# Query tiles from the last to the first in a fused attention, mixture and gating kernel

## The chip, the cores and the metric

The kernel runs on one core of a Trainium2 chip. The metric is the device time of one execution in microseconds (us). PE is TensorE, DVE is VectorE, ACT is ScalarE, POOL is GpSimd, SP issues the DMAs.

## The reference

Eight batches of 576 rows. A linear attention with a normalisation gives x (576 x 512); then four experts of causal attention (head size 64), each weighted by a top-2 gate; then a gated MLP that mixes along the sequence.

```python
kv = einsum('bhsd,bhse->bhde', k, v)              # "kv"
out = einsum('bhsd,bhde->bhse', q, kv)            # "o", then / rms * g_norm -> x
q, k, v = x @ wq[e], x @ wk[e], x @ wv[e]         # "qk", "v"
a = softmax(causal(scale * q @ k.T))              # "s", "exp", "scale"
x2 = sum over the chosen e of w_e * (a @ v @ wo[e])   # "t", "pv"
h = gelu(x2 @ w_in);  u, v = halves of h          # "u", "h"
v_s = w_sg @ layernorm(v) * g_ln + b_sg           # "vs"
y = x2 + (u * v_s) @ w_out                        # "out"
```

## The kernel before

Every engine walks one list, PLAN[part], and does its share of each unit (kind, j) in that order. There is no scheduler: the order of the lists is the order on each engine. Part -1 prepares weights and x of batch 0; parts 0 to 7 each do a batch, with the first product (kv, qT, o, x) of the next batch inside. Part 0 also splits the weights into a high and a low half (kinds split, w2e, wsgT, wsgR, wout).

The 640 rows (576 and 64 of padding) are five tiles of 128. An attention step n is one query tile and one pair of experts: tile n // 2, pair n % 2, ten steps. A step is

- s: PE scores (scores, L905 on), to a wide PSUM slot (w0, w1), 64 to 576 keys; step tiles of 576 keys take both slots. Two maxima by DVE (maximum, L695) follow.
- exp: two exponentials by ACT (L581), one for each expert of the pair.
- scale: DVE (scale_probs, L701) takes row_eps, row_inv and multiplies probs, and takes the maxima of the next step in between.
- t, t2: PE transposes probs to the narrow slots t0, t1 (L941), ACT copies them to work (L596); of a tile of five key blocks the last two (t2) are copied by DVE (L837).
- pv: PE multiplies with vals (L957) to a slot of t2, t3; when the second pair is in, ACT copies the tile's result to yT (L600) and DVE makes its low half (L829).

A unit waits on PE until the slot's last user is drained (dst). qk and v units are 12 matmuls of a projection (split_product, L887): the copy of a qk unit goes through ACT (L565) and then DVE (L815), and only then is the slot drained. scores asks for the drained qk units of its queries and keys. v units are copied by ACT (L561). h is 6 matmuls; gelu on ACT (L608), the statistics (L732), normalise (L742) and vhat_low (L727) on DVE, ln_inv on POOL and vhat_high (L524) on ACT make the layer norm, five tiles in turn. u units (L887, copied by a gelu, L610) go to w0, w1, w0, w1 and ask for all of yT; vs needs all five vhat tiles.

Of the kernel before, what the change touches and what calls it, by code (L numbers as in the profile page):

```python
# [55 lines left out]
def moe_chain(nc, q, k, v, g_norm, w_gate, wq, wk, wv, wo, w_in, g_ln, w_sg, b_sg, w_out, out):  # L56
# [18 lines left out]
    QK_ORDER = (0, EP, 1, EP + 1)  # L75
# [5 lines left out]
              ("split", "wqk0"), ("o", 3), ("x", 1), ("split", "wqk2"), ("w2", 3), ("o", 4), ("x", 2), ("x", 3), ("x", 4)]  # L81
# [13 lines left out]
    def attention(late_qk, late):  # L95

        plan = []
        for m in QK_ORDER:
            plan += [("qk", (m, 0))] + late_qk.get(m, [])
        for n in range(N - 2):  # L100
            plan += [("s", n)] + [("scale", n - 1)] * (n >= 1) + [("t", n - 2)] * (n >= 2) + [("exp", n)]
            plan += (late.get(n, []) if n == 0 else []) + BETWEEN.get(n, []) + (late.get(n, []) if n > 0 else [])
            plan += [("pv", n - 3)] * (n >= 3)
        return plan + [("t", N - 4), ("scale", N - 3), ("s", N - 2), ("exp", N - 2), ("pv", N - 5), ("t", N - 3),
                       ("pv", N - 4), ("scale", N - 2), ("s", N - 1), ("exp", N - 1)]

    ATTENTION = attention({}, {})
# [5 lines left out]
    MLP += [("u", m) for m in range(FC)] + [("vs", m) for m in range(FC)]  # L113

# [3 lines left out]
    GATE_STEP = [1, 8]  # L118
# [18 lines left out]
    def score_slots(n):  # L137

        return [(("s", n), WIDE[n % 2])] if P * (n // 2 + 1) - PAD <= 512 else [(("s", n, a), WIDE[a]) for a in range(2)]

    def scores_at(n, a):

        K = P * (n // 2 + 1) - PAD
        units_ = score_slots(n)
        unit, slot = units_[a % len(units_)]
        return unit, slot, 512 * a if len(units_) == 1 else W_LO, K

    def units(part):

        turn, got = [ring_start(part)], []  # L150

        def ring(unit, among):
            if part < 0:
                got.append((unit, FIRST_SLOT[unit]))
                return
            got.append((unit, among[turn[0] % len(among)]))
            turn[0] += 1

        for kind, j in PLAN[part]:
            if kind == "s":  # L160
                got += score_slots(j)
            elif kind == "t":
                got += [(("t", j, a, 0), NARROW[a]) for a in range(2)]
            elif kind == "t2":
                got += [(("t", j, a, 1), NARROW[a]) for a in range(2)]
            elif kind == "pv":
                if j % 2 == 0:
                    ring(("y", j // 2), NARROW[2:])
            elif kind in ("split", "double", "exp", "scale", "gelu", "wout", "w2e"):
                pass  # L170
            elif kind == "w2":
                if j == 0:
                    got += [((kind, c), WIDE[c]) for c in range(EP)]
            elif kind == "kv":
                if j == 0:
                    ring(("kv", 0), NARROW[2:])
            elif kind in ("u", "vs", "woT"):
                got.append(((kind, j), WIDE[j % 2]))
            elif kind == "out_y":
                got.append((("out", j), WIDE[j % 2]))  # L180
            elif kind == "out_g":
                pass
            elif kind == "h" and j in H_SLOT:
                got.append(((kind, j), H_SLOT[j]))
            elif kind in ("v", "h", "wsgT", "wsgR") or (kind == "qk" and j[1] == 1):
                ring((kind, j), NARROW[2:])
            else:
                ring((kind, j), NARROW)
        return got

    with ExitStack() as ctx:
# [319 lines left out]
        def _(act):  # L511
            def body(part):
# [8 lines left out]
                def vhat_high(s):  # L521
                    act.wait_ge(ln_ready, count(part, NT, s + 1))
                    rows = slice(PAD if s == 0 else 0, P)
                    nc.scalar.activation(vhat[rows, HI, s, :], ln_tile[s % 2][rows, :], ACT.Copy).then_inc(vhat_hi, 1)  # L524

                for kind, j in PLAN[part]:
# [40 lines left out]
                    elif kind == "s":  # L567
                        for g, (lo, hi) in enumerate(GATES):
                            if j == GATE_STEP[g]:
                                act.wait_ge(gate_dif, count(part, 2, g + 1))  # L570
                                nc.scalar.activation(g_exp[:, lo:hi, :], g_dif[:, lo:hi, :], ACT.Exp).then_inc(gate_exp, 1)
                    elif kind == "exp":
                        if j >= 2:

                            for a in range(2):
                                u.wait_full(act, part, ("t", j - 2, a, 0))
# [8 lines left out]
                    elif kind == "t":  # L585
                        lo, hi = T_GROUPS[j // 2][0]
# [11 lines left out]
                    elif kind == "pv" and j % 2 == 1:  # L598
                        t = j // 2
# [28 lines left out]
        def _(dve):  # L628
# [4 lines left out]
            def body(part):  # L633
# [18 lines left out]
                def gate_ranks(lo, hi):  # L652
# [3 lines left out]
                    u.wait_drained(dve, part, ("v", hi - 1))  # L656
# [44 lines left out]
                def scale_probs(n, maxima_of=None):  # L701

                    t, e = n // 2, n % 2
                    for g, (lo, hi) in enumerate(GATES):
                        if t == lo and e == 0:
                            gate_weights(g, lo, hi)
# [16 lines left out]
                def vhat_low(s):  # L723
                    dve.wait_ge(vhat_hi, count(part, NT, s + 1))

                    rows, dst = (slice(PAD, P), vhat[0:PAD, HI, 0, :]) if s == 0 else (slice(0, P), vhat[:, LO, s, :])
                    nc.vector.tensor_tensor(dst, ln_tile[s % 2][rows, :], as_f32(vhat[rows, HI, s, :]),  # L727
# [23 lines left out]
                for kind, j in PLAN[part]:  # L751
# [55 lines left out]
                    elif kind == "v":  # L807
                        for lo, hi in GATES:
                            if j == hi - 1:
                                gate_ranks(lo, hi)  # L810
# [8 lines left out]
                    elif kind == "s":  # L819
                        if not 2 <= j < N - 2:  # L820
                            maximum(j, 0)
                            maximum(j, 1)
                    elif kind == "scale":
                        scale_probs(j, j + 1 if 2 <= j + 1 < N - 2 else None)
                    elif kind == "pv":
                        if j % 2 == 1:
                            t = j // 2
                            dve.wait_ge(yT_hi, count(part, NT, t + 1))
# [4 lines left out]
                    elif kind == "t2":  # L833
                        lo, hi = T_GROUPS[j // 2][1]
# [35 lines left out]
        def _(pe):  # L870
            def body(part):
# [25 lines left out]
                def scores(n):  # L897
                    t, e = n // 2, n % 2

                    last_col = P * (t + 1)  # L900
                    u.wait_drained(pe, part, ("qk", (e, int(last_col > PAD + HALF))))
# [43 lines left out]
                def weighted_values(n):  # L945

                    t, e = n // 2, n % 2
# [15 lines left out]
                for kind, j in PLAN[part]:  # L963
# [34 lines left out]
                    elif kind == "wsgT":  # L998
                        if j == 0:
                            pe.wait_ge(wsg_doubled, 1)  # L1000
# [4 lines left out]
                    elif kind == "wsgR":  # L1005
                        x = dst(U)
# [43 lines left out]
                    elif kind == "qk":  # L1050
# [4 lines left out]
                        if part == 0:  # L1055
                            pe.wait_ge(wqk_lo, QK_ORDER.index(m) + 1)
# [8 lines left out]
                    elif kind == "h":  # L1065

                        u.wait_drained(pe, part, ("y", j))
                        finish(split_product([dst(U)[:, 0:512]], lambda h, c: yT[:, h, c, P * j:P * (j + 1)],
                                             [lambda h, c: w2_s[:, h, c, FF:2 * FF]], range(EP)), U)
                    elif kind == "u":  # L1070

                        u.wait_drained(pe, part, ("y", NT - 1))
                        finish(split_product(both_banks(dst(U)), lambda h, c: w2_s[:, h, c, P * j:P * (j + 1)],
                                             both_halves(yT, PAD), range(EP)), U)
                    elif kind == "vs":

                        outs = both_banks(dst(U))
                        if j == 0:
# [3 lines left out]
                            pe.wait_ge(vhat_lo, count(part, NT, 1))  # L1082
                        for h in (HI, LO):
                            for r, o in enumerate(outs):
                                nc.tensor.matmul(o, vhat[:, HI, 0, P * j:P * (j + 1)],  # L1085
                                                 wsgT_s[:, h, 0, HALF * r:HALF * (r + 1)], start=h == HI, stop=False)
                        finish(split_product(outs, lambda h, c: vhat[:, h, c, P * j:P * (j + 1)], both_halves(wsgT_s, 0),
                                             range(1, NT), of=range(NT),
                                             ready=lambda c: pe.wait_ge(vhat_lo, count(part, NT, c + 1)) if j == 0 else None), U)
# [43 lines left out]
```

## Time and profile before

| what | us |
|---|---|
| median of 3 runs | 914.76 (911.61 to 914.87) |
| the profiled execution | 911.67 |
| its span, first to last instruction | 909.9 |
| PE busy | 878.0 |
| DVE, ACT, POOL busy | 459.7, 410.6, 181.5 |

Parts 1 to 6 take 107.8 to 107.95 us each. PE is the engine that is hardly ever idle; what matters for a change of order is how long PE stands still, and what it then waits for. Matmuls overlap, so the pace of a unit is read from its start to the start of the next.

### The profile page before, as it was taken

The page shows a single profiled execution, that of the slowest core. Times are in us where ns is not written, and L with a number is a line of the kernel's source. Part 1 is how long each engine was busy: PE and PEld are TensorE (multiplying, and loading weights), DVE is VectorE, ACT ScalarE, POOL GpSimd, SP SyncE. Part 2 cuts the span into 40 slices and gives each one's busy share as a digit, 9 for nine tenths or more (in the row PEclk, how much of TensorE's full clock was granted, in tenths as well). Part 3 has the DMA queues.
Part 4 walks back from the last instruction along what each step waited for, and adds up shares of the span by engine and source line. Part 5 has one row for each costly group of instructions (what it writes and reads, how often), then busy time and mean ns, then how long its engine had stood idle before and what let it go on. Part 6 is the DMA issues. An engine that isn't in the chain of part 4 may idle for free.

```text
span 909.9 us, 17540 instructions
## 1 busy us (share of the span) xinstructions
PE 878.0 (96%) x7009; PEld 764.5 (84%) x7009; DVE 459.7 (51%) x1221; ACT 410.6 (45%) x978; POOL 181.5 (20%) x213
## 2 busy tenths in 40 slices
PE   6898999999999999999999999999999999999898
PEld 4686898979988798977989789897998879897796
DVE  1567723475345743377334772347534674337730
ACT  1457523474335633465244652347433563336521
POOL 0402233002420034101330023300342003410130
PEclk9999999999999999999999999999999999999999
DMA  9902313003030032100330030300303000000001
GB/s 278 233 1 67 108 36 93 12 2 105 6 99 1 1 106 58 49 1 8 99 82 24 1 82 25 93 12 2 106 7 99 2 2 1 23 31 1 1 1 53
DMA packets 77648, 45.76 MB, mean 50 GB/s; under 512 B 54592, under 2 KB 70976, under 8 KB 77568
## 3 DMA queue, kind: packets, MB, share of 16 engines
q1 hardware_dynamic: 77568, 44.63, 18.6%
q8 instruction: 57, 0.93, 0.4%
q14 instruction: 23, 0.19, 0.1%
HBM read 35.19 MB, written 9.44 MB: 49 GB/s over the span
## 4 chain that ended last, share of the span: by engine, by line
PE 79%; DVE 9%; ACT 8%; SPq 2%; issue 1%; DMA 1%; POOL 0%; POOLq 0%; ACTq 0%; DVEq 0%
PE w L887 38%; PE t L887 19%; ACT probs L581 5%; PE t L941 4%; PE t L1033 4%; PE w L926 3%; DVE neg_max L698 3%; PE t L957 3%; DVE probs L719 2%; PE t L1022 2%; PE w L1085 2%; PE t L1041 2%; PE t L973 2%; ACT work L596 1%; DVE yT L829 1%
## 5 line engine op out<-in xcount | busy, mean ns | idle before, releaser
L887 PE MATMUL w<-wout_s,big 128*128 128x512 f32 x480 | 119.2, 397 | 1.6 <-DVE big L747 1.6
L887 PE MATMUL t<-big,wqk_s 128*128 128x288 f32 x768 | 111.4, 301 | 0.9 <-DVE big L815 0.6
L887 PEld LDWEIGHTS w<-wout_s,big 128*128 128x128 f32 x480 | 89.3, 188 | 22.0 <-DVE big L747 2.1
L887 PE MATMUL w<-wsgT_s,big 128*128 128x288 f32 x768 | 107.7, 296 | 0.0
L887 PEld LDWEIGHTS t<-big,wqk_s 128*128 128x128 f32 x768 | 104.4, 190 | 1.8 <-issue 1.5
L887 PEld LDWEIGHTS w<-wsgT_s,big 128*128 128x128 f32 x768 | 104.3, 189 | 0.0
L581 ACT ACTIVATE probs<-w,neg_max 128x64 f32<-128x64 f32 (+4 forms) x160 | 83.0, 526 | 46.6 <-DVE neg_max L698 43.6
L497 POOL TENSOR_TENSOR var_eps<-bn,eps_t 128x1 f32<-128x1 f32 x40 | 13.3, 333 | 415.4 <-DVE bn L735 414.7
L596 ACT ACTIVATE work<-t 128x384 f32<-128x384 f32 (+3 forms) x160 | 63.1, 450 | 44.5 <-PE t L941 42.7
L941 PE MATMUL t<-ident,probs 128*128 128x128 f32 x480 | 72.5, 282 | 8.0 <-DVE probs L719 6.9
L620 ACT ACTIVATE work<-w 128x512 f32<-128x512 f32 x40 | 23.9, 597 | 118.9 <-PE w L887 118.9
L504 POOL TENSOR_TENSOR work<-work,qT_uT 128x576 f32<-128x576 f32 x32 | 54.7, 1709 | 113.6 <-DVE work L856 113.6
L856 DVE SCALAR_TENSOR_TENSOR work<-w,gln_c,bias_t 128x576 f32<-128x576 f32 x32 | 26.2, 818 | 99.5 <-PE w L887 99.5
L614 ACT ACTIVATE big<-work 128x576 fp32r<-128x576 f32 x32 | 21.9, 686 | 120.7 <-POOL work L504 120.7
L698 DVE TENSOR_REDUCE neg_max<-w 128x1 f32<-128x64 f32 (+4 forms) x160 | 73.9, 483 | 4.5 <-PE w L926 3.4
L941 PEld LDWEIGHTS t<-ident,probs 128*128 128x128 f32 x480 | 52.0, 140 | 27.4 <-DVE probs L719 16.8
L957 PE MATMUL t<-work,vals 128*64 128x128 f32 x960 | 70.1, 281 | 2.2 <-DVE work L837 0.8
L792 DVE TENSOR_REDUCE ss<-squares 128x8 f32<-128x512 f32 x40 | 27.4, 686 | 86.1 <-ACT squares L553 86.1
L474 POOL TENSOR_TENSOR rms_inv<-ms,neg_half 128x8 f32<-128x8 f32 x40 | 65.6, 1641 | 3.1
L719 DVE TENSOR_SCALAR probs<-probs,row_inv,gate 128x64 f32<-128x64 f32 (+4 forms) x160 | 64.2, 443 | 2.9
L957 PEld LDWEIGHTS t<-work,vals 128*64 128x64 f32 x960 | 51.0, 136 | 16.5 <-issue 13.2
L926 PE MATMUL w<-big 64*128 64x288 f32 (+4 forms) x576 | 64.2, 328 | 0.0
(106 smaller groups left out, 1414.0 us busy)
## 6 DMA issues: line engine op xcount, KB each, us to landing
kin<-in_k_dram SPq DMA_DIRECT2D x8, 1024.0 KB, 6.3
vin<-in_v_dram SPq DMA_DIRECT2D x8, 1024.0 KB, 8.8
qin<-in_q_dram SPq DMA_DIRECT2D x32, 256.0 KB, 4.8
out_dram<-work SPq DMA_DIRECT2D x32, 256.0 KB, 2.1
staged_win<-in_moe_w_in_dram SPq DMA_DIRECT2D x4, 512.0 KB, 5.3
staged<-in_moe_w_sg_dram SPq DMA_DIRECT2D x4, 288.0 KB, 3.8
kin<-in_k_dram SPq DMA_DIRECT2D x8, 128.0 KB, 2.8
vin<-in_v_dram SPq DMA_DIRECT2D x8, 128.0 KB, 7.0
```

What stands on the lines that cost most here:

```text
L474: nc.gpsimd.tensor_tensor(rms_inv[:, j, :], ms[:, j, :], neg_half[:, 0:H], ALU.pow).then_inc(rms_ready, 1)
L504: nc.gpsimd.tensor_tensor(gt_tile[j % 2], gt_tile[j % 2], qT_uT[:, j, PAD:SP], ALU.mult).then_inc(gated_ready, 1)
L581: exps = nc.scalar.activation(probs[:, j % 2, a, PAD:PAD + K], ps[slot][:, o:o + K], ACT.Exp, bias=neg_max[:, j, a:a + 1], accum_out=row_s ...
L596: give(nc.scalar.activation(pT[:, j % 2, a, P * lo:P * hi], x[:, 0:P * (hi - lo)], ACT.Copy), V)
L698: nc.vector.tensor_reduce(neg_max[:, n, a:a + 1], ps[slot][:, o:o + K], AX_X, ALU.max, negate=True).then_inc(max_ready, 1)
L719: last = nc.vector.tensor_scalar(x, x, row_inv[:, n, a:a + 1], gate[:, t, 2 * e + a:2 * e + a + 1], ALU.mult, ALU.mult)
L792: nc.vector.tensor_reduce(ss[:, j, :], sq_tile.rearrange("p (h d) -> p h d", h=H), AX_X, ALU.add).then_inc(ss_ready, 1)
L887: last = nc.tensor.matmul(o, stationary(hs, c), mv(hm, c), start=c == of[0] and p == 0, stop=c == of[-1] and p == len(PASSES) - 1)
L926: last = nc.tensor.matmul(ps[slot][:, o:o + w], big2[rows, hs, e, P * t:P * (t + 1)], big2[rows, hm, EP + e, PAD + k0:PAD + k0 + w], start ...
L941: last = nc.tensor.transpose(x[:, P * (b - lo):P * (b - lo + 1)], probs[:, n % 2, a, P * b:P * (b + 1)], ident[:, :])
L957: last = nc.tensor.matmul(x[HD * a:HD * (a + 1), P * e:P * (e + 1)], vals[:, b, w:w + HD], pT[:, n % 2, a, P * b:P * (b + 1)], start=b == ...
L1033: last = nc.tensor.matmul(x[:, P * c:P * (c + 1)], qT_uT[:, c, P * j:P * (j + 1)], kvd[:, c, :], start=True, stop=True)
```

## The change

Step n now belongs to tile 4 - n // 2: the longest steps come first, the shortest last. Projections (qk, v) stand beside the first steps, kv of the next batch beside steps 6 and 7 (in part 0 after the last gelu), the h units after the last step. The layer norm runs in the order of tiles 4 to 0, and vs takes its chunks so. GATES is turned, and the exponential of the gate is a unit of its own (gexp). exp of step n now waits for all transposes of step n - 2. In part 0 the splits of weights are placed anew.

```diff
+    def tile(n):
+        return NT - 1 - n // 2
...
-    BETWEEN = {0: [("v", t) for t in range(4)], 1: [("qk", (0, 1)), ("qk", (EP, 1))], 2: [("qk", (1, 1))],
-               3: [("qk", (EP + 1, 1))], 7: [("v", 4)]}
-    GATES = [(0, 4), (4, NT)]
+    BETWEEN = {0: [("v", 4), ("qk", (1, 1)), ("gexp", 0), ("qk", (EP + 1, 1))], 1: [("v", 3), ("v", 2)],
+               2: [("v", 1), ("t2", 0), ("v", 0), ("gexp", 1)], 3: [("qk", (0, 0)), ("t2", 1)], 4: [("qk", (1, 0))]}
+    GATES = [(4, NT), (0, 4)]
+    def attention(early, late):
+        plan = [("qk", (EP, 0)), ("qk", (EP + 1, 0)), ("qk", (0, 1)), ("qk", (EP, 1))]
+        for n in range(N):
+            plan += [("scale", 0), ("s", 1)] if n == 1 else [("s", n)] + [("scale", n - 1)] * (n >= 2)
+            plan += [("t", n - 2)] * (n >= 2) + [("exp", n)] + BETWEEN.get(n, []) + early.get(n, [])
             plan += [("pv", n - 3)] * (n >= 3)
+    ATTENTION = attention({6: KV[:2], 7: KV[2:]}, {})
...
-    MLP = [("pv", N - 3), ("t", N - 2), ("h", 0), ("h", 1), ("scale", N - 1), ("t2", N - 2), ("gelu", 0), ("gelu", 1),
-           ("h", 2), ("pv", N - 2), ("t", N - 1), ("h", 3), ("t2", N - 1), ("gelu", 2), ("kv", 0), ("pv", N - 1),
-           ("gelu", 3)] + [("kv", c) for c in range(1, DC)] + [("h", 4), ("gelu", 4)]
+    MLP = [("t", N - 2), ("pv", N - 3), ("scale", N - 1), ("h", 0), ("t", N - 1), ("pv", N - 2), ("h", 1), ("pv", N - 1),
+           ("gelu", 0), ("h", 2), ("gelu", 1), ("h", 3), ("gelu", 2), ("h", 4), ("gelu", 3), ("gelu", 4)]
...
-                            for a in range(2):
-                                u.wait_full(act, part, ("t", j - 2, a, 0))
+                            for g in range(len(T_GROUPS[tile(j - 2)])):
+                                for a in range(2):
+                                    u.wait_full(act, part, ("t", j - 2, a, g))
```

Lines of the changed kernel are 4 to 9 higher than before. On PE, at the start of batch 1, the four qk units (48 matmuls) are followed before the change by the first score step and by four v units (L919 is the causal mask, L926 the scores):

```order
L1041 MATMUL t<-ident,work 128x128 x4
L887 MATMUL t<-big,wqk_s 128x288 x48
L919 MATMUL w<-causal,ident_h 128x64 x2
L926 MATMUL w<-big 128x64 x6
L887 MATMUL t<-wv_s,big 128x260 x48
L919 MATMUL w<-causal,ident_h 128x64 x2
L926 MATMUL w<-big 128x64 x6
L887 MATMUL t<-big,wqk_s 128x288 x24
```

In the changed kernel they are followed by the longest score step, one v unit, two qk units and the second score step (L924 the mask, L931 the scores):

```order
L892 MATMUL t<-big,wqk_s 128x288 x48
L931 MATMUL w<-big 128x288 x6
L924 MATMUL w<-causal,ident_h 128x128 x2
L931 MATMUL w<-big 128x288 x6
L892 MATMUL t<-wv_s,big 128x260 x12
L892 MATMUL t<-big,wqk_s 128x288 x24
L931 MATMUL w<-big 128x288 x6
L924 MATMUL w<-causal,ident_h 128x128 x2
L931 MATMUL w<-big 128x288 x6
```

Both long score steps now stand directly behind the qk units from which they read, with no unit between.

On PE, from the second h unit (L887 with w_s; the first stands one row ahead) to the u units (L887 with 128x288 into w), before:

```order
L887 MATMUL w<-w_s,yT 128x512 x6
L941 MATMUL t<-ident,probs 128x128 x4
L887 MATMUL t<-w_s,yT 128x512 x6
L957 MATMUL t<-work,vals 64x128 x10
L941 MATMUL t<-ident,probs 128x128 x6
L887 MATMUL w<-w_s,yT 128x512 x6
L941 MATMUL t<-ident,probs 128x128 x4
L1022 MATMUL t<-vin,kin 64x64 x10
L957 MATMUL t<-work,vals 64x128 x10
L1022 MATMUL t<-vin,kin 64x64 x30
L887 MATMUL t<-w_s,yT 128x512 x6
L887 MATMUL w<-yT,w_s 128x288 x48
```

And after, from the last score step on (L946 transposes, L962 the product with vals, L892 with w_s the h units and then the u units):

```order
L931 MATMUL w<-big 128x64 x6
L946 MATMUL t<-ident,probs 128x128 x4
L962 MATMUL t<-work,vals 64x128 x4
L946 MATMUL t<-ident,probs 128x128 x2
L962 MATMUL t<-work,vals 64x128 x4
L892 MATMUL w<-w_s,yT 128x512 x6
L946 MATMUL t<-ident,probs 128x128 x2
L962 MATMUL t<-work,vals 64x128 x2
L892 MATMUL w<-w_s,yT 128x512 x6
L962 MATMUL t<-work,vals 64x128 x2
L892 MATMUL t<-w_s,yT 128x512 x18
L892 MATMUL w<-yT,w_s 128x288 x48
```

The h units moved from between the last steps to behind them, and the kv product (L1022, L1026) away from them.

On ACT, from the first gelu on, before (L608 gelu, L524 the high half of the layer norm, L600 yT, L610 the gelu of u):

```order
L608 ACT_TABLE_LOAD
L608 ACTIVATE staged<-t 128x512
L608 ACTIVATE staged<-w 128x512
L596 ACTIVATE work<-t 128x384 x2
L608 ACTIVATE staged<-t 128x512
L524 ACTIVATE big<-staged 64x512
L600 ACTIVATE yT<-t 128x2x128
L608 ACTIVATE staged<-w 128x512
L524 ACTIVATE big<-staged 128x512
L608 ACTIVATE staged<-t 128x512
L524 ACTIVATE big<-staged 128x512
L610 ACTIVATE qT_uT<-w 128x576
```

And after (L612, L528, L604, L614):

```order
L600 ACTIVATE work<-t 128x128 x2
L604 ACTIVATE yT<-t 128x2x128
L612 ACT_TABLE_LOAD
L612 ACTIVATE staged<-w 128x512 x2
L612 ACTIVATE staged<-t 128x512
L528 ACTIVATE big<-staged 128x512
L612 ACTIVATE staged<-t 128x512
L528 ACTIVATE big<-staged 128x512
L612 ACTIVATE staged<-t 128x512
L528 ACTIVATE big<-staged 128x512
L614 ACTIVATE qT_uT<-w 128x576
```

All copies of probs and yT now stand ahead of the table load, and of the first gelu.

## Rows read from the trace of the kernel before

Times are us from the start of the span. A row of the timeline is start, duration, engine, line, operation, tiles, count.

**Rows 1.** The page: engine, busy us (share), instructions.

```profile
PE 878.0 (96%) x7009; PEld 764.5 (84%) x7009; DVE 459.7 (51%) x1221; ACT 410.6 (45%) x978; POOL 181.5 (20%) x213
```

**Rows 2.** Windows: length, busy us of each engine, clock: 1st, 2nd, last.

```profile
50.90:158.67 107.77, 103.08 (x837) 89.83 (x838) 60.95 (x155) 52.68 (x126) 26.72 (x28) 1.00 0.24 65
158.67:266.55 107.88, 106.61 (x871) 93.99 (x870) 55.58 (x150) 49.96 (x121) 21.63 (x24) 1.00 0.17 45
...
806.00:909.90 103.90, 95.89 (x711) 82.61 (x709) 45.49 (x134) 42.73 (x107) 12.41 (x14) 1.00 0.04 15
```

**Rows 3.** Timeline of PE, batch 1: start, us, what, [idle before].

```profile
186.72 0.87 PE L941 MATMUL t<-ident,probs 128*128 128x128 f32 x6 [0.54 <-DVE probs L719]
...
200.47 0.88 PE L941 MATMUL t<-ident,probs 128*128 128x128 f32 x6 [0.32 <-DVE probs L719]
...
202.89 1.63 PE L887 MATMUL w<-w_s,yT 128*128 128x512 f32 x6 [0.16 <-ACT probs L581]
```

**Rows 4.** Waits of PE, last batch: us in total, times, longest.

```profile
PE t L887 <- DVE yT L829: 1.0, 1, 1.0
...
PE t L957 <- DVE work L837: 0.8, 1, 0.8
```

**Rows 5.** Timeline of PE, batch 1: units at their pace.

```profile
165.08 0.23 PE L919 MATMUL w<-causal,ident_h 128*128 128x64 bf16 x2
...
183.19 0.71 PE L926 MATMUL w<-big 64*128 64x320 f32 x6
...
192.37 1.09 PE L941 MATMUL t<-ident,probs 128*128 128x128 f32 x8
...
206.28 1.31 PE L957 MATMUL t<-work,vals 128*64 128x128 f32 x20
...
215.55 6.56 PE L887 MATMUL w<-yT,w_s 128*128 128x288 f32 x48
```

**Rows 6.** Timeline of ACT, batch 1.

```profile
165.27 0.41 ACT L565 ACTIVATE big<-t 128x288 fp32r<-128x288 f32 x1 [1.17 <-PE t L887]
...
193.06 1.08 ACT L596 ACTIVATE work<-t 128x512 f32<-128x512 f32 x2 [0.66 <-PE t L941]
...
203.80 1.28 ACT L608 ACT_TABLE_LOAD   x1
205.09 0.60 ACT L608 ACTIVATE staged<-t 128x512 f32<-128x512 f32 x1
```

**Rows 7.** Timeline of DVE, batch 1.

```profile
165.71 0.46 DVE L815 SCALAR_TENSOR_TENSOR big<-t,big 128x288 fp32r<-128x288 f32 x1 [1.12 <-ACT big L565]
...
205.72 0.69 DVE L732 BATCH_NORM_STATS2 bn<-staged 128x6 f32<-128x512 f32 x1 [0.19 <-ACT staged L608]
...
206.66 0.66 DVE L732 BATCH_NORM_STATS2 bn<-staged 128x6 f32<-128x512 f32 x1
...
207.68 0.55 DVE L742 TENSOR_SCALAR staged<-staged,bn,ln_inv 128x512 f32<-128x512 f32 x1
```

**Rows 8.** Groups by shape, ACT: busy us, mean ns | idle before.

```profile
L610 ACT ACTIVATE qT_uT<-w 128x576 f32<-128x576 f32 x32 | 20.9, 653 | 17.3 <-PE w L887 17.3
L524 ACT ACTIVATE big<-staged 128x512 fp32r<-128x512 f32 x32 | 20.1, 630 | 0.2
L581 ACT ACTIVATE probs<-w,neg_max 128x448 f32<-128x448 f32 x32 | 20.1, 635 | 2.0 <-DVE neg_max L698 2.0
...
L600 ACT ACTIVATE yT<-t 128x256 fp32r<-128x256 f32 x40 | 15.5, 389 | 18.4 <-PE t L957 18.4
```

**Rows 9.** Groups by shape, DVE.

```profile
L727 DVE TENSOR_TENSOR big<-staged,big 128x512 fp32r<-128x512 f32 x32 | 22.0, 686 | 0.8
...
L829 DVE TENSOR_TENSOR yT<-t,yT 128x256 fp32r<-128x256 f32 x40 | 17.0, 425 | 33.0 <-ACT yT L600 32.5
...
L711 DVE TENSOR_SCALAR row_eps<-row_sum 128x2 f32<-128x2 f32 x80 | 13.7, 172 | 0.8
...
L719 DVE TENSOR_SCALAR probs<-probs,row_inv,gate 128x64 f32<-128x64 f32 x32 | 8.6, 311 | 0.6
```

More of the change, by code:

```diff
@@ L107, in moe_chain @@
-    ATTENTION = attention({}, {})
-    MLP = [("pv", N - 3), ("t", N - 2), ("h", 0), ("h", 1), ("scale", N - 1), ("t2", N - 2), ("gelu", 0), ("gelu", 1),
-           ("h", 2), ("pv", N - 2), ("t", N - 1), ("h", 3), ("t2", N - 1), ("gelu", 2), ("kv", 0), ("pv", N - 1),
-           ("gelu", 3)] + [("kv", c) for c in range(1, DC)] + [("h", 4), ("gelu", 4)]
-    MLP += [("u", m) for m in range(FC)] + [("vs", m) for m in range(FC)]
+    LATE = {("qk", (EP, 0)): [("split", "wqk0"), ("w2e", 0)], ("qk", (EP + 1, 0)): [("w2e", 1)],
+            ("qk", (0, 1)): [("split", "wv")], ("exp", 0): [("split", "wqk1")],
+            ("exp", 1): [("double", 0), ("split", "wo")], ("exp", 3): [("wsgR", 0), ("wout", 0)],
+            ("exp", 4): [("wsgT", 0), ("wout", 1)], ("exp", 5): [("wsgT", 1), ("wout", 2)],
+            ("exp", 6): [("wsgT", 2), ("wout", 3)], ("exp", 7): [("wsgT", 3)], ("exp", 8): [("wsgT", 4)]}
@@ L137, in score_slots @@
     def score_slots(n):
-        return [(("s", n), WIDE[n % 2])] if P * (n // 2 + 1) - PAD <= 512 else [(("s", n, a), WIDE[a]) for a in range(2)]
+        return [(("s", n), WIDE[n % 2])] if P * (tile(n) + 1) - PAD <= 512 else [(("s", n, a), WIDE[a]) for a in range(2)]
     def scores_at(n, a):
-        K = P * (n // 2 + 1) - PAD
+        K = P * (tile(n) + 1) - PAD
         units_ = score_slots(n)
@@ L167, in units @@
                 if j % 2 == 0:
-                    ring(("y", j // 2), NARROW[2:])
-            elif kind in ("split", "double", "exp", "scale", "gelu", "wout", "w2e"):
+                    ring(("y", tile(j)), NARROW[2:])
+            elif kind in ("split", "double", "exp", "scale", "gelu", "wout", "w2e", "gexp"):
                 pass
@@ L522, in vhat_high @@
                     act.wait_ge(ln_ready, count(part, NT, s + 1))
-                    rows = slice(PAD if s == 0 else 0, P)
-                    nc.scalar.activation(vhat[rows, HI, s, :], ln_tile[s % 2][rows, :], ACT.Copy).then_inc(vhat_hi, 1)
+                    rows = slice(PAD if s == NT - 1 else 0, P)
+                    nc.scalar.activation(vhat[rows, HI, NT - 1 - s, :], ln_tile[s % 2][rows, :], ACT.Copy).then_inc(vhat_hi, 1)
                 for kind, j in PLAN[part]:
@@ L701, in scale_probs @@
                 def scale_probs(n, maxima_of=None):
-                    t, e = n // 2, n % 2
+                    t, e = tile(n), n % 2
                     for g, (lo, hi) in enumerate(GATES):
-                        if t == lo and e == 0:
+                        if t == hi - 1 and e == 0:
                             gate_weights(g, lo, hi)
@@ L724, in vhat_low @@
                     dve.wait_ge(vhat_hi, count(part, NT, s + 1))
[L726 to L727 removed]
+                    t = NT - 1 - s
+                    rows, dst = (slice(PAD, P), vhat[0:PAD, HI, 0, :]) if t == 0 else (slice(0, P), vhat[:, LO, t, :])
+                    nc.vector.tensor_tensor(dst, ln_tile[s % 2][rows, :], as_f32(vhat[rows, HI, t, :]),
                                             ALU.subtract).then_inc(vhat_lo, 1)
@@ L1081, in body @@
                                     u.wait_drained(pe, part, unit)
-                            pe.wait_ge(vhat_lo, count(part, NT, 1))
+                        split_product(outs, lambda h, c: vhat[:, h, c, P * j:P * (j + 1)], both_halves(wsgT_s, 0),
+                                      range(NT - 1, 0, -1), of=range(NT - 1, -1, -1),
+                                      ready=lambda c: pe.wait_ge(vhat_lo, count(part, NT, NT - c)) if j == 0 else None)
+                        if j == 0:
+                            pe.wait_ge(vhat_lo, count(part, NT, NT))
                         for h in (HI, LO):
                             for r, o in enumerate(outs):
[L1085 to L1089, printed above, removed]
+                                last = nc.tensor.matmul(o, vhat[:, HI, 0, P * j:P * (j + 1)],
+                                                        wsgT_s[:, h, 0, HALF * r:HALF * (r + 1)], start=False, stop=h == LO)
+                        finish(last, U)
                     elif kind == "out_y":
```

74 lines of the change are left out of this document (32 added, 42 removed).

## The prediction, made before the changed kernel ran

> **What bounds the kernel now.** I first read how much of the span each engine works: PE is busy for 878.0 of 909.9 us, DVE for 459.7 [rows 1]. Then the windows: in batch 1 PE works 106.61 of 107.88 us at a granted clock of 1.00; batches 2 to 6 look the same. The window of batch 0 has 103.08 of 107.77 us, that of the last batch 95.89 of 103.90 [rows 2]. So PE sets the time, and all that a change of order can give is PE's idle time: 1.3 us in each of six batches, 4.7 in batch 0, and a few in the last. The timeline of PE names it: in batch 1 it waits three times, 0.54, 0.32 and 0.16 us, 1.0 in all, for scaled probs and for the slot of an exponential [rows 3]. In the last batch, which has no kv product to do beside them, the h units and the last pv wait too, 1.0 and 0.8 us [rows 4]. The change moves work and adds none: PE's matmuls are the same in number and shape. The question is then only where the new order makes PE stand still.
>
> **The two score steps behind their projections.** scores asks for drained qk units. Before, step 0 needs the first two of four units, so two units of cover lie between. Now step 0 (tile 4) needs the third and the fourth and stands right behind the fourth; step 1 needs the two units of pair 1 and stands right behind the second. What a drain takes is in the trace: PE could issue its next unit at 165.08 [rows 5], ACT copied the last qk unit from 165.27 [rows 6], DVE made the low half from 165.71 for 0.46 us [rows 7], so it was drained at 166.17. With a few hundredths for the semaphore that is 1.1 us of PE idle, with nothing else to issue. The table load for the exponential lies beside it. Twice: **2.2 us a batch**. Step 1 cannot be later than that by DVE: the gate's ranks, about 1.0 us of small operations, end before the second copy comes. Bound from below: 1.0 each, from above 1.5 each if DVE is busy with the gate.
>
> **Steps 3 and 4.** The transposes of step 2 use slots t0 and t1 after t2 of step 1, which DVE copies, behind the low half of qk (0, 0), which ACT copies behind exp 3, and exp 3 now waits for t2 of step 1. From the end of that t2 the chain is: 0.13 to reach ACT, two exponentials of 448 columns 1.2 (635 ns each [rows 8]), ACT's copy 0.44 to the start of DVE's low half (165.27 to 165.71), 0.38 for that low half less its overlap with what follows, and DVE's first copy, 0.46 if it is like a low half [rows 6, 7]: 2.6 us. PE has meanwhile a pv unit of 20 matmuls (1.31, or 1.25 to the next) and a score unit of 320 columns (0.71 and its mask pair ahead, 0.9) [rows 5]: 2.2. Wait: **0.4**. Then qk (1, 0) falls on slot t1, which the same transposes have just filled. They took 1.09 from 192.37 [rows 5], ACT's two copies 1.08 from 193.06 [rows 6]: the slot was free at 194.14 and PE at 193.46. Wait: **0.7**. 0 and 0.9 bound each of them.
>
> **The last steps.** Before, the last steps are long ones and their chains run beside h and pv. Now, with nothing but short units left, t of step 8 waits for a chain: pv 5, ACT's yT copy 389 ns [rows 8], DVE's low half 425 ns, maxima, row_eps 172 ns and row_inv, two multiplications of 311 ns [rows 9], since DVE takes them in that order. With 0.2 to leave PE and the overlaps this is about 2.2 us against 1.8 of PE (s 9, t 7, pv 6). t of step 9 waits for the same chain behind pv 7, some 1.9 us, with one h unit of 1.5 beside it [rows 3]. Wait: **0.4 each**, bounds 0 and 0.9.
>
> **The layer norm.** This is the dearest. Before, the table load for gelu starts at 203.80 and the first gelu at 205.09 [rows 6], 10.5 us ahead of the u units at 215.55 [rows 5]: two more t, two pv, three h and the kv product lie between. Now ACT comes to it only behind the yT copy of pv 9, and PE has three h units (4.6 us) and then u 0 and u 1 (6.4 / 4 each, 3.2) until u 2 needs the slot of u 0. Count from the end of pv 9 on PE: 0.2, yT copy 0.39, table load 1.28 [rows 6], gelu 0.60 and 0.03: statistics start at 2.5. From there DVE's order binds. Statistics 0 to normalise 0 took 1.96 (205.72 to 207.68), one statistics 0.94 (205.72 to 206.66), a normalise gives way after 0.46 [rows 7] and a vhat_low (686 ns [rows 9]) after 0.6. So: normalise 0 at 1.96, statistics 2, normalise 1 at 3.4, vhat_low 0, statistics 3, normalise 2 at 5.4, done at 6.0. ACT has vhat_high 2 (630 ns) ahead of the gelu of u 0 (653 ns [rows 8]): drained at 7.2, so 9.7 after pv 9. PE is there at 7.8. Wait for u 0's slot: **1.9 us**; then u 1's behind vhat_high 3: **0.4**. vs finds its vhat tiles just in time. Bounds: 1.2, if the gelus begin earlier than this, and 3, if POOL's ln_inv is slower beside a busy DVE.
>
> The Trainium skill bears on the table load here. The row shows 1.28 us of load, with the gelu 0.01 behind it [rows 6]. "ScalarE: Activation LUTs", section "What ACT_TABLE_LOAD costs", puts a drain of about 1.38 us beside each load, 2.66 in all. By the row the wait is 1.9; by the page it would be about 3.3.
>
> **The sum.** New waits of a batch: 2.2 + 0.4 + 0.7 + 0.8 + 1.9 + 0.4 = 6.4. The old ones, 1.0, go. Net 5.4, times six batches: 32.4. The last batch gets the same 6.4 and perhaps 0.5 for the kv that no longer covers steps 6 and 7, and loses its own 1.0 and 0.8 besides the 1.0 of every batch: +4. In batch 0 the kv product stands behind the gelus and covers the layer norm's 2.3, but splits are in the way. A split is a copy by ACT and one by DVE of the shapes of vhat (0.63 and 0.69 [rows 8, 9]): qk (0, 1) waits 0.3 for its weights, s 0 one us more behind a full DVE, qk (1, 1) 2.3 for a split that ACT takes only behind exp 0, and with weights to copy in every step some 3 us more: 11 against 4.7 idle now [rows 2]. +6. Together 42.4, on the profiled execution's 911.67 (span 909.9, 1.8 around it): 954. The median of the runs, 914.76, is 3.1 above that execution and the lowest run is level with it; I put 955.
>
> **The rivals.** (1) Only the firm waits stay, those that one chain fixes (2.2 and 2.3); the soft ones of steps 3, 4, 8 and 9 hide, since every earlier wait gives DVE and ACT time: 1.9 less in eight batches and 1 in batch 0, 939. For it: DVE is busy for half the time [rows 1]. Chance 0.17.
> (2) Queues add up: soft waits at their upper bounds (0.9 four times, 1.7 more a batch), 968. For it: ACT and DVE take everything in list order. Chance 0.19.
> (3) Other side: the exchange pays. Before, the wait for probs at 186.72 [rows 3] comes from steps that have only short PE units beside them; if projections beside the long steps hide all that, and new waits of a batch come to 0.5, the kernel gains 0.5 eight times and some 2 us of batch 0: 906. It decides at 1.0 of new waits a batch; the two waits behind qk alone are 2.2. Chance 0.02.
> (4) The switch to gelu is dearer where nothing hides it, 1.4 us in seven batches: 965. It was not so at 203.80. Chance 0.04. That is the skill's figure above.
> (5) The clock. Waits of up to 1.0 us in the last batch left it at 1.00 [rows 2, 4]. If a 1.9 us wait sends it to the 1.2 GHz level during the u units (6.4 us at 2.4 GHz), each batch loses 6 more: about 1000. Chance 0.03. "TensorE: Matmul & The Clock Gate" of the Trainium skill warns, under "Why this matters for your kernels", of idle gaps between bursts of matmuls; no gap of this trace inside a batch shows it.
>
> **How the numbers follow.** My own case has 0.55 and lies between 946 and 963. The range takes in most of rivals 1, 2 and 4: 936 to 971. Slower by over 0.5% (which is about what a measurement of this kernel can tell from no change) in all cases but rival 3 and a remainder: 0.97; same 0.01; faster 0.02.
>
> **What will show it.** The PE timeline of a middle batch should have a wait of 1.1 for the low half of a qk unit (DVE L820) ahead of each of the two first score steps, one of about 1.9 ahead of the third u unit for a gelu of ACT, and small ones for probs and for slots t0, t1. The batch should take 113 us instead of 107.9. PE's busy time should stay within 2 of 878. Two waits behind qk that are missing, or an idle time below 4 us a batch, would prove me wrong; so would a clock below 1.

## The result: 5.9% slower

| | before | changed |
|---|---|---|
| median | 913.18 us (911.07 to 914.87, 4 runs) | 966.04 us (964.83 to 969.76, 4 runs) |
| profiled execution, its span | 911.67, 909.9 | 969.76, 968.0 |

The ratio is 1.059 (1.056 to 1.062). The forecast was 955 with a range of 936 to 971: the sign and the size are right, and so is the mechanism but for one wait, that of score step 4. 11 us are missing from the sum.

The page of the changed kernel, beside [rows 1]:

```profile
PE 894.1 (92%) x7009; PEld 773.0 (80%) x7009; DVE 459.0 (47%) x1221; ACT 409.3 (42%) x978; POOL 180.4 (19%) x213
```

The other engines do the same work as before. PE has the same 7009 matmuls, but 16 us more busy time, and 42 us more of idle time (73.9 against 31.9, span less busy). The sum of the prediction was one of idle time alone, 42.4 us; its sign that PE's busy time stays within 2 us of 878 failed. The windows of batch 1, of batch 3 and of the last batch (length, busy time of each engine, clock) answer to [rows 2]:

```profile
169.62:284.93 115.31, 108.83 (x872) 95.53 (x870) 55.58 (x150) 49.77 (x121) 21.50 (x24) 0.99 0.16 42
400.09:514.43 114.34, 107.67 (x871) 94.08 (x870) 55.58 (x150) 49.76 (x121) 21.50 (x24) 1.00 0.16 42
859.56:968.00 108.44, 97.05 (x711) 82.87 (x709) 45.40 (x134) 42.44 (x107) 12.29 (x14) 1.00 0.04 14
```

Batches 1 to 6 are of two kinds: two take 114.34 us at a clock of 1.00, four take 115.16 to 115.46 at 0.99, all instead of 107.88. The timeline of PE in batch 1 (the waits in brackets) shows where they go; before, it had the three waits of [rows 3]:

```profile
177.26 0.66 PE L931 MATMUL w<-big 64*128 64x288 f32 x6 [1.04 <-issue]
...
184.61 0.67 PE L931 MATMUL w<-big 64*128 64x288 f32 x6 [1.04 <-issue]
...
200.37 0.28 PE L924 MATMUL w<-causal,ident_h 128*128 128x128 bf16 x2 [1.14 <-DVE big L820]
...
203.14 1.82 PE L892 MATMUL t<-big,wqk_s 128*128 128x288 f32 x12 [0.83 <-ACT work L600]
...
220.37 0.44 PE L946 MATMUL t<-ident,probs 128*128 128x128 f32 x2 [0.23 <-DVE probs L723]
...
223.19 0.44 PE L946 MATMUL t<-ident,probs 128*128 128x128 f32 x2 [0.21 <-DVE probs L723]
...
235.54 4.94 PE L892 MATMUL w<-yT,w_s 128*128 128x288 f32 x24 [2.00 <-ACT qT_uT L614]
```

The reader is to see seven waits, in the order of the prediction: scores 0, scores 1, scores 4, the slot of qk (1, 0), t 8, t 9, and u 2, whose slot u 0's gelu has to leave. They add up to 6.49 us. For the first two the profile finds no releaser and says "issue"; that they are waits for drained qk units is read from the code of scores, and two experiments below test it. The three old waits are gone. The last row also shows something else: 24 matmuls in 4.94 us, where the 24 of u 0 and u 1 took 3.36.

The list of PE's waits over the whole span (total, times, longest) says that the other batches have them too, but for batch 0, which lacks those of scores 4 and u 2:

```profile
PE w L931 <- issue: 16.9, 16, 1.3
PE w L892 <- ACT qT_uT L614: 14.6, 10, 2.0
PE w L924 <- DVE big L820: 8.0, 7, 1.1
PE t L892 <- ACT work L600: 6.2, 8, 0.8
...
PE t L946 <- DVE probs L723: 3.6, 16, 0.3
```

The difference of the two profiled executions, 58.1 us, splits by where the batches begin: 4.6 before batch 0 (mostly DMAs of q and v that came later; PE waited 1.6 us for q before, 4.0 for q and 1.0 for v now, and 0.6 to 3.0 for q in the profiled executions of the other kernels, so I do not count it to the change), 6.4 in batch 0, 42.6 in batches 1 to 6, 4.5 in the last.

### The profile page after: what moved, and what is told of

The parts are those of the page before. It is cut to its first block, busy times and chain, and to the rows that moved or that the text cites. A ratio compares the mean times of both kernels' runs of the same rounds, so it can differ in the third digit from the quotient of the medians.

```text
span 968.0 us, 17556 instructions
## 1 busy us (share of the span) xinstructions
PE 894.1 (92%) x7009; PEld 773.0 (80%) x7009; DVE 459.0 (47%) x1221; ACT 409.3 (42%) x978; POOL 180.4 (19%) x213
## 4 chain that ended last, share of the span: by engine, by line
PE 77%; DVE 8%; ACT 8%; issue 4%; SPq 2%; POOL 1%; DMA 1%; POOLq 0%; DVEq 0%; ACTq 0%
PE w L892 32%; PE t L892 17%; PE t L946 6%; PE w L931 6%; PE t L962 4%; PE t L1037 4%; DVE bn L737 2%; PE w L1094 2%; ACT probs L585 2%; PE t L1045 2%; PE t L978 2%; PE t L1026 2%; DVE staged L747 2%; ACT work L600 2%; PE w L924 1%
## 5 line engine op out<-in xcount | busy, mean ns | idle before, releaser
L892 PE MATMUL w<-wout_s,big 128*128 128x512 f32 x480 | 119.2, 397 | 1.6 <-DVE big L752 1.6
L892 PE MATMUL t<-big,wqk_s 128*128 128x288 f32 x768 | 112.0, 302 | 8.5 <-ACT work L600 6.2
L892 PEld LDWEIGHTS t<-big,wqk_s 128*128 128x128 f32 x768 | 105.6, 192 | 10.8 <-ACT work L600 7.9
L585 ACT ACTIVATE probs<-w,neg_max 128x576 f32<-128x576 f32 (+4 forms) x160 | 83.1, 530 | 68.2 <-DVE neg_max L702 43.3
L892 PE MATMUL w<-wsgT_s,big 128*128 128x288 f32 x768 | 107.6, 296 | 0.1
L892 PEld LDWEIGHTS w<-wout_s,big 128*128 128x128 f32 x480 | 89.3, 188 | 22.0 <-DVE big L752 2.1
L892 PEld LDWEIGHTS w<-wsgT_s,big 128*128 128x128 f32 x768 | 103.8, 189 | 0.6 <-ACT qT_uT L614 0.3
L702 DVE TENSOR_REDUCE neg_max<-w 128x1 f32<-128x576 f32 (+4 forms) x160 | 75.3, 485 | 39.5 <-PE w L931 39.1
L600 ACT ACTIVATE work<-t 128x384 f32<-128x384 f32 (+3 forms) x160 | 63.0, 446 | 73.2 <-PE t L946 70.5
L931 PE MATMUL w<-big 64*128 64x288 f32 (+4 forms) x576 | 64.1, 327 | 16.9 <-issue 16.9
L946 PE MATMUL t<-ident,probs 128*128 128x128 f32 x480 | 72.7, 282 | 3.6 <-DVE probs L723 3.6
L892 PE MATMUL w<-yT,w_s 128*128 128x288 f32 x384 | 61.3, 319 | 14.6 <-ACT qT_uT L614 14.6
L892 PEld LDWEIGHTS w<-yT,w_s 128*128 128x128 f32 x384 | 58.0, 208 | 17.9 <-issue 17.2
L962 PE MATMUL t<-work,vals 128*64 128x128 f32 x960 | 69.5, 280 | 2.4 <-DVE wsgT_s L792 2.4
L946 PEld LDWEIGHTS t<-ident,probs 128*128 128x128 f32 x480 | 51.6, 140 | 19.4 <-DVE probs L723 9.0
```

The source lines that it names most:

```text
L585: exps = nc.scalar.activation(probs[:, j % 2, a, PAD:PAD + K], ps[slot][:, o:o + K], ACT.Exp, bias=neg_max[:, j, a:a + 1], accum_out=row_s ...
L600: give(nc.scalar.activation(pT[:, j % 2, a, P * lo:P * hi], x[:, 0:P * (hi - lo)], ACT.Copy), V)
L702: nc.vector.tensor_reduce(neg_max[:, n, a:a + 1], ps[slot][:, o:o + K], AX_X, ALU.max, negate=True).then_inc(max_ready, 1)
L892: last = nc.tensor.matmul(o, stationary(hs, c), mv(hm, c), start=c == of[0] and p == 0, stop=c == of[-1] and p == len(PASSES) - 1)
L931: last = nc.tensor.matmul(ps[slot][:, o:o + w], big2[rows, hs, e, P * t:P * (t + 1)], big2[rows, hm, EP + e, PAD + k0:PAD + k0 + w], start ...
L946: last = nc.tensor.transpose(x[:, P * (b - lo):P * (b - lo + 1)], probs[:, n % 2, a, P * b:P * (b + 1)], ident[:, :])
```

## The experiments

Each starts from the changed kernel, if not said otherwise. Medians; "a batch" is one of batches 1 to 6 without a fall of the clock, 114.34 us in the changed kernel. The changed kernel was not measured again beside the experiments; the kernel before was, with medians of 912.38 and 911.85, so a gain against the changed kernel's 966.04 is uncertain by a microsecond or so (an estimate from these medians and 913.18).

### kv back behind the gelus

```diff
-    ATTENTION = attention({6: KV[:2], 7: KV[2:]}, {})
+    ATTENTION = attention({}, {})
...
-    PLAN.update({b: ATTENTION + MLP + MIXED for b in range(1, B - 1)})
+    PLAN.update({b: ATTENTION + MLP_FIRST + MIXED for b in range(1, B - 1)})
```

> The kv product of the next batch goes back behind the last gelu in batches 1 to 6 (2.5 us of matmuls between h and u), nothing else is changed. Changed kernel: 966 us. Theory A (the 2.0 us wait for the slot of u 0 is the layer norm's chain, and the slow u units behind it, 4.8 instead of 3.2 us, are the clock that falls because of that wait): both go in six batches, 3.4 us each, 20 in all: 946. Rival B (kv beside steps 6 and 7 was needed there: their short units now wait for probs, some 1 us a batch): 952. Rival C (the clock falls whether or not PE waits): only the wait goes, 954.

Measured: 951.14 us (ratio to before 1.043, 1.040 to 1.046). The waits in its trace, whole span, without the rows of the start:

```profile
PE w L931 <- issue: 17.1, 16, 1.6
PE w L924 <- DVE big L820: 8.0, 7, 1.1
PE t L892 <- ACT work L600: 6.2, 8, 0.8
...
PE t L946 <- DVE probs L723: 3.6, 16, 0.3
...
PE w L892 <- ACT qT_uT L614: 2.2, 2, 2.0
```

The wait for u 0's slot is left only in the last batch, which has no kv. The waits for probs are 3.6 us in 16, as in the changed kernel: kv covered nothing at steps 6 and 7, so rival B falls. All of batches 1 to 6 have a clock of 1.00 and take 112.30 to 112.49, 2.0 less than the better kind: rival C falls too. That the gain is 15 and not 20 comes from the clock: it fell in four of the six batches and cost 1.0 us each time, where I had put 1.4 in every one (below).

### The gelu of u ahead of the layer norm's high half

```diff
-    VHAT_AFTER = {("gelu", 2): 0, ("gelu", 3): 1, ("gelu", 4): 2, ("u", 0): 3, ("u", 1): 4}
+    VHAT_AFTER = {("gelu", 2): 0, ("gelu", 3): 1, ("u", 0): 2, ("u", 1): 3, ("u", 2): 4}
```

> On ACT the gelu of u 0 stands ahead of the third high half of the layer norm, and so for u 1 and u 2; kv stays at steps 6 and 7. Theory A (the wait of 2.0 us for u 0's slot comes from its place in ACT's list, behind a high half that waits for DVE): the wait and the fall of the clock behind it go, 3.4 us in most of seven batches: 944, if the layer norm is done in time for vs. Rival B (the layer norm itself is the bound: u runs through and vs waits for its vhat tiles instead, 1 to 2 us): 952 to 960.

Measured: 949.89 us (1.042, 1.039 to 1.045); a batch 112.56. On PE, batch 1:

```profile
233.77 3.43 PE L892 MATMUL w<-yT,w_s 128*128 128x288 f32 x24 [0.50 <-ACT qT_uT L614]
```

The wait is 0.50 instead of 2.00, and no batch has slow u units. vs does not wait, so rival B is not what is left; the 0.5 is the gelu of u 0 behind gelu 4. The wait of 2 us came from the place of u 0's gelu in ACT's list, behind a high half that itself waits for the layer norm on DVE. Two quite different edits that take away the same wait, this one without moving any matmul, both take the fall of the clock with it.

### A v unit as cover ahead of the first two score steps

```diff
-        plan = [("qk", (EP, 0)), ("qk", (EP + 1, 0)), ("qk", (0, 1)), ("qk", (EP, 1))]
+        plan = [("qk", (EP, 0)), ("qk", (EP + 1, 0)), ("qk", (0, 1)), ("qk", (EP, 1)), ("v", 4)]
...
-    BETWEEN = {0: [("v", 4), ("qk", (1, 1)), ("gexp", 0), ("qk", (EP + 1, 1))], 1: [("v", 3), ("v", 2)],
+    BETWEEN = {0: [("qk", (1, 1)), ("gexp", 0), ("qk", (EP + 1, 1)), ("v", 3)], 1: [("v", 2)],
```

> One v unit (1.5 us) is put between the qk units and each of the first two score steps: v 4 ahead of step 0, v 3 ahead of step 1. Theory A (the two waits of 1.04 us are the drain of the last qk unit and nothing else): 2.08 in eight batches, 16.6 less, 949.5; no wait ahead of the scores of steps 0 and 1. Rival B (DVE, which also has the gate's ranks and the first long probs, is the real limit, and the wait turns up again at step 1 or at the transposes of step 0): 958 to 966.

Measured: 954.56 us (1.047, 1.045 to 1.049); a batch 112.76. Both waits of 1.04 are gone. A small one is new, two units later, where score step 2 needs a slot that an exponential has not left:

```profile
183.66 0.27 PE L924 MATMUL w<-causal,ident_h 128*128 128x128 bf16 x2 [0.27 <-ACT probs L585]
```

2.08 gone and 0.27 new make 1.81; the batch is 1.58 shorter. So the waits were the drains, as theory A says, but of its 16.6 us only 11.5 came in the medians. In the profiled executions batch 0 gained nothing (124.85 us against 123.31), and a new small wait turned up at step 2, where B had looked one step too early.

### qk (0, 0) and qk (1, 0) earlier

```diff
-               2: [("v", 1), ("t2", 0), ("v", 0), ("gexp", 1)], 3: [("qk", (0, 0)), ("t2", 1)], 4: [("qk", (1, 0))]}
+               2: [("v", 1), ("t2", 0), ("v", 0), ("gexp", 1), ("qk", (0, 0))], 3: [("qk", (1, 0)), ("t2", 1)]}
...
-            elif kind in ("v", "h", "wsgT", "wsgR") or (kind == "qk" and j[1] == 1):
+            elif kind in ("v", "h", "wsgT", "wsgR") or (kind == "qk" and (j[1] == 1 or j[0] < EP)):
```

> qk (0, 0) stands behind v 0 instead of in step 3, qk (1, 0) in step 3 instead of 4, and both use slots t2 and t3. Theory A (the score step 4 waits 1.14 us for the drained qk (0, 0), whose copy stands behind exp 3, and qk (1, 0) waits 0.83 for slot t1): both waits go; the transposes of step 2 may then wait some 0.4 for the slots that DVE's t2 copies hold: 1.6 less in eight batches, 953. Rival B (the chain exp 3, copies, transposes of step 2 is late by itself and takes the place of both): 962 or more.

Measured: 961.43 us (1.054, 1.051 to 1.057); a batch 113.57, only 0.8 less. PE, batch 2:

```profile
306.98 1.81 PE L892 MATMUL t<-big,wqk_s 128*128 128x288 f32 x12 [0.51 <-ACT vals L565]
...
315.37 1.06 PE L946 MATMUL t<-ident,probs 128*128 128x128 f32 x8 [0.71 <-DVE work L842]
```

The two waits are gone as A says, 1.97 us, and two others came: qk (0, 0) for the slot of v 1, whose copy stands behind exp 2, and the transposes of step 2 for the slots that DVE's t2 copies hold, 0.71 where 0.4 was expected. So B is nearer: by these rows ACT and DVE are late in this stretch whichever unit asks for them. No run makes that chain shorter by itself.

### qk (1, 0) in another slot

```diff
-            elif kind in ("v", "h", "wsgT", "wsgR") or (kind == "qk" and j[1] == 1):
+            elif kind in ("v", "h", "wsgT", "wsgR") or (kind == "qk" and (j[1] == 1 or (part > 0 and j[0] < EP))):
```

> qk (1, 0) gets slot t3 instead of t1 in batches 1 to 7; the order is untouched. Theory A (it waits 0.83 us only for ACT's copy of the transposes that lie in t1): that wait goes in seven batches, 5.8 less than the changed kernel's 966: 960. Rival B (the transposes of step 3, the next in the list, then wait for the same copies): 965.

Measured: 955.76 us (1.048, 1.046 to 1.049); a batch 113.28. The wait of 0.83 is gone from all seven batches and nothing came in its place (the next transposes start without one), so A holds for the cause, and the batch is 1.06 shorter, more than the wait in the row. Seven times 1.06 are 7.4 of the 10.3 us in the median; in the profiled executions four of the changed kernel's batches fell back to the lower clock and two here, which is 2 more.

### Three edits together

kv behind the gelus, the cover, and the early qk units.

> The three edits of the first experiments together: kv behind the gelus, a v unit ahead of each of the first two score steps, qk (0, 0) and (1, 0) earlier. Each of them alone left 951, 954.6 and 961.4 us of the changed kernel's 966. Theory A (the waits are separate terms of one sum): the gains of 15, 11.5 and 4.5 add up to 31: 935. Rival B (they share a chain, so that one edit's gain is another's): 943 or more. Rival C (with all of them gone the order that starts with the long steps beats the one before): under 912.

Measured: 937.48 us (1.028, 1.027 to 1.029); a batch 109.93. Alone the edits took 2.04, 1.58 and 0.77 off a batch, 4.39; together 4.41. In a batch at full clock the terms are separate, and their sum is exact to 0.02 us. The 935 by medians missed by 2.5: batch 0 took 127.10 us in the profiled execution against 123.31 in the changed kernel. What stands against 107.88 before is, first, five waits left:

```profile
296.06 0.27 PE L924 MATMUL w<-causal,ident_h 128*128 128x128 bf16 x2 [0.25 <-ACT probs L585]
301.78 1.81 PE L892 MATMUL t<-big,wqk_s 128*128 128x288 f32 x12 [0.51 <-ACT vals L565]
310.16 1.06 PE L946 MATMUL t<-ident,probs 128*128 128x128 f32 x8 [0.71 <-DVE work L842]
324.30 0.44 PE L946 MATMUL t<-ident,probs 128*128 128x128 f32 x2 [0.24 <-DVE probs L723]
327.12 0.44 PE L946 MATMUL t<-ident,probs 128*128 128x128 f32 x2 [0.21 <-DVE probs L723]
```

1.92 us, against the old 1.02. Besides, PE is busy for 107.89 us in this batch against 106.61 before, which no row of waits explains (below). Rival C falls: this order with these bare spots covered is still slower.

### The kernel before, with its first score step behind its projection

```diff
-    QK_ORDER = (0, EP, 1, EP + 1)
+    QK_ORDER = (1, EP + 1, 0, EP)
```

and the splits of part 0 in the same order.

> The kernel before, with one thing changed: the four qk units of a batch in the order (1, 0), (3, 0), (0, 0), (2, 0), so that score step 0 stands directly behind the unit it reads (splits of part 0 follow that order). Theory A (a score step right behind its projection costs the whole way through ACT and DVE, about 1.04 us, whatever else is in the kernel): 8 us more, 921. Rival B (the wait only shows in the new order, where DVE and ACT are late): 913.

Measured: 922.05 us (1.012, 1.010 to 1.014), 10.2 more than the 911.85 of the kernel before; a batch 109.07 instead of 107.88. PE, batch 2:

```profile
275.29 0.22 PE L919 MATMUL w<-causal,ident_h 128*128 128x64 bf16 x2 [1.04 <-issue]
```

The same 1.04 us appears in a kernel whose DVE and ACT are not late. That shows the cause of the first two waits by itself: two pairs of units swapped, no work moved past another stage. The batch is 1.19 longer for a row of 1.04.

### The kernel before, with pv 3 ahead of t 4

```diff
-            plan += [("s", n)] + [("scale", n - 1)] * (n >= 1) + [("t", n - 2)] * (n >= 2) + [("exp", n)]
+            early_pv = [("pv", n - 3)] * (n == 6)
+            plan += [("s", n)] + [("scale", n - 1)] * (n >= 1) + early_pv + [("t", n - 2)] * (n >= 2) + [("exp", n)]
...
-            plan += [("pv", n - 3)] * (n >= 3)
+            plan += [("pv", n - 3)] * (n >= 3 and n != 6)
```

> The kernel before, with pv 3 ahead of t 4 in step 6, so that PE has the 0.6 us of pv to do while it waits 0.54 us for scaled probs. Theory A (the wait is cover that was missing, and goes): 4 us less in eight batches, 908.5. Rival B (the same chain is late again a step later, since nothing on DVE got faster, and the yT copy now stands ahead of the exponentials): 912 to 914.

Measured: 908.53 us (907.37 to 911.86, 9 runs), ratio 0.9967 (0.9951 to 0.9982): 3.3 us or 0.3% less than the 911.85 of the kernel before, measured beside it; small, but clear of the interval. Theory A had promised 4. A batch takes 107.32 instead of 107.88. The wait of 0.54 [rows 3] has gone, one of 0.26 came a step later, as rival B said in kind, and the other two are as before:

```profile
295.66 0.88 PE L942 MATMUL t<-ident,probs 128*128 128x128 f32 x6 [0.26 <-DVE probs L720]
306.80 0.87 PE L942 MATMUL t<-ident,probs 128*128 128x128 f32 x6 [0.32 <-DVE probs L720]
309.22 1.63 PE L888 MATMUL w<-w_s,yT 128*128 128x512 f32 x6 [0.16 <-ACT probs L582]
```

## Why the prediction was right, and what its sum missed

**The two score steps behind their projections.** Predicted 1.1 each, measured 1.04 each in every batch. Shown by the cover (gone) and by the kernel before with the pairs swapped (there). 1.1 was right because the whole way was read from rows: ACT's copy, DVE's low half, the semaphores.

**Steps 3 and 4.** Here a step of the prediction failed. I put 0.4 on the transposes of step 2 waiting for their slots. The wait is 1.14 and stands one unit earlier: score step 4 reads the queries of qk (0, 0), a dependence I had passed over, though scores asks for it in plain words. That the wait comes from this dependence is shown by the early qk units, which take it away. The chain is the one I had priced, but PE has less beside it. The copies of ACT and DVE ahead of it in batch 1:

```profile
198.18 0.63 ACT L585 ACTIVATE probs<-w,neg_max 128x448 f32<-128x448 f32 x1 [1.64 <-PE t L946]
...
198.81 0.62 ACT L585 ACTIVATE probs<-w,neg_max 128x448 f32<-128x448 f32 x1
...
199.42 0.41 ACT L569 ACTIVATE big<-t 128x288 fp32r<-128x288 f32 x1
```

```profile
199.85 0.46 DVE L820 SCALAR_TENSOR_TENSOR big<-t,big 128x288 fp32r<-128x288 f32 x1 [0.50 <-ACT big L569]
```

The low half ends at 200.31, PE goes on at 200.37, and only the pv unit lay beside the chain. By the early qk units, the slot wait I had named appears too (0.71) once the dependence is out of the way. The slot of qk (1, 0): predicted 0.7, measured 0.83, and 1.06 by the experiment that frees it.

**The last steps.** Predicted 0.4 each, measured 0.23 and 0.21: mis-sized. At t 8 the chain took 2.09 us and not 2.2 (from the end of pv 5 at 218.28 to 220.37), and at t 9 PE's h unit covered 1.66 and not 1.5.

**The layer norm.** Predicted 1.9 for u 0's slot, measured 2.00; for u 1's, 0.4 predicted and 0.18 measured in a batch at full clock. What ACT and DVE did, in batch 1:

```profile
226.40 1.28 ACT L612 ACT_TABLE_LOAD   x1
227.70 1.09 ACT L612 ACTIVATE staged<-w 128x512 f32<-128x512 f32 x2
...
234.23 0.63 ACT L528 ACTIVATE big<-staged 128x512 fp32r<-128x512 f32 x1 [0.89 <-DVE staged L747]
234.77 0.63 ACT L614 ACTIVATE qT_uT<-w 128x576 f32<-128x576 f32 x1
```

This is the chain as it was walked. The table load takes 1.28 us and the gelu follows 0.02 after it; rival 4, the dearer switch, did not come. The drain of 1.38 us that the Trainium skill ("ScalarE: Activation LUTs", "What ACT_TABLE_LOAD costs") adds to a switch is not seen in this trace, here as little as before.

**Batch 0 and the last.** 6 and 4 predicted, 6.4 and 4.5 measured; in batch 0 that is partly luck. PE's idle time there rose by 3.6 us only (8.6 against 5.0), and its busy time by 2.75, with one more fall of the clock behind a wait of 2.08 us. In the last batch idle rose by 3.4 and busy by 1.2.

**The clock.** Rival 5 had the right mechanism, a chance that was too small (0.03) and a price that was too large (6 us a batch). A clock below 1 was one of the signs that were to prove me wrong, and it came, in four batches. Windows of one microsecond in batch 1 (length, PE, PEld, DVE, ACT, POOL busy, clock):

```profile
234.00:235.00 1.00, 0.00 (x0) 0.00 (x0) 1.00 (x3) 0.77 (x2) 0.92 (x2) 1.00 0.00 0
235.00:236.00 1.00, 0.46 (x3) 0.49 (x4) 0.85 (x3) 0.40 (x1) 0.38 (x2) 1.00 0.00 0
236.00:237.00 1.00, 1.00 (x8) 1.00 (x7) 0.81 (x2) 0.76 (x2) 0.92 (x2) 0.65 0.00 0
237.00:238.00 1.00, 1.00 (x6) 1.00 (x6) 0.68 (x2) 0.52 (x2) 0.20 (x1) 0.50 0.00 0
238.00:239.00 1.00, 1.00 (x6) 1.00 (x6) 0.91 (x2) 0.97 (x2) 0.00 (x0) 0.50 0.08 16
239.00:240.00 1.00, 1.00 (x7) 1.00 (x6) 0.24 (x1) 0.20 (x1) 0.00 (x0) 0.64 0.00 0
```

PE stood still until 235.54; about 0.8 us later, when it was at work again, the granted clock fell to 0.50, the 1.2 GHz level, for 3.4 us and came back. It cost about 1.0 us of the batch (115.31 against 114.34), since the slow u 2 hides the wait for u 1's slot. It happened behind four of the seven waits of 2.0 us in the changed kernel, and behind none of the waits of 0.5 us when the gelu of u went first.

**The sum.** Predicted net 5.4 a batch, measured 6.46 at full clock. PE's idle time in such a batch rose from 1.27 to 6.67, which is 5.40: the forecast to the digit, and that is luck, since 0.7 too little at score step 4 is made up by the last steps, by u 1 and by short old idle times that I had not counted. The other 1.06 stands in no row of waits: PE's busy time in the window rose from 106.61 to 107.67. The prediction put that term at nothing, because the matmuls are the same. Part of it belongs to the waits. The start of batch 1 shows how:

```profile
169.62 6.60 PE L892 MATMUL t<-big,wqk_s 128*128 128x288 f32 x48
```

Before, the same 48 matmuls led to the next unit after 6.41 us (158.67 to 165.08); now it starts after 7.64 (177.26). The wait cost 1.23, its row says 1.04: the last matmul ahead of a wait is counted as busy to its end, which otherwise lies under the next one. So too freeing one slot gave 0.2 more than its row. The rest of the 1.06 was not separated. Six times 1.06, four falls of the clock and 0.9 in the first and last batches make 11, which is what the medians miss (966 against 955). Of the 42.0 us of idle time, 3.4 lie before batch 0, where the DMAs came later, so that the match with 42.4 for the whole span is in part luck as well.

## What to carry to other kernels

When every engine walks one list, a reordering is priced by asking of each unit on the busiest engine what lies between it and the last thing it reads, all the way through the copies, and of each copy what stands ahead of it in its own engine's list. Read those dependences from the code for every unit that moved; the durations of the old trace then gave all the waits here but one to about 0.2 us, and by the three edits together they add up. The one that was missed was a dependence not read. The rows are not quite the price either: rows of 1.04 and 0.83 us were worth 1.19 and 1.06, the cover's 1.81 only 1.58. Here a unit of independent work between producer and consumer took away the whole wait; putting the long steps first gained nothing that the runs show.

## What the runs showed that I had not expected

A wait of 2.0 us in the midst of dense matmuls was sometimes enough for the clock to fall, and sometimes not: by the pace of the u units behind it, in four of seven batches of the changed kernel, in three of seven with the cover, in four of seven with the early qk units, in two of seven with the other slot. Behind the one wait of 2.0 us that is left with kv behind the gelus, and with the three edits together, it did not fall. What decides is not known. Waits of 1.0 to 1.14 us between long stretches of work showed no fall in batches 1 to 6. But in the last batch of the kernel with the swapped pairs it fell (0.57 in the window 869 to 873) right behind two such waits close together:

```profile
866.93 1.31 PE L957 MATMUL t<-work,vals 128*64 128x128 f32 x20 [0.83 <-DVE work L837]
869.26 2.93 PE L887 MATMUL t<-w_s,yT 128*128 128x512 f32 x6 [1.02 <-DVE yT L829]
```

The kernel before has the same two waits, and its clock stayed up there in the profiled execution. Two kernels with the same list of waits can so differ by some us, and one kernel from run to run. "TensorE: Matmul & The Clock Gate" of the Trainium skill warns, under "Why this matters for your kernels", that idle gaps between bursts of matmuls bring the lower clock. The trace agrees in kind, 0.50 behind a gap of 2.0 us; but the gap that the page names is longer, and the traces show a shorter one to be enough at times.

A wait can be wider than its row: the slot experiment took away a row of 0.83 us and gave back 1.06, and the swapped pairs brought one of 1.04 and cost 1.19.
